# Other shares of the stores of output chunks 0 to 2 among the DMA engines

## The reference, cut to what matters

```python
kv = einsum('bhsd,bhse->bhde', k, v); out = einsum('bhsd,bhde->bhse', q, kv)
x = out / sqrt(mean(out * out, -1) + 1e-06) * g_norm      # -> 4608 tokens x 512
logits = x @ phi                                          # 4608 x 32 slots
d = softmax(logits over tokens); slot_input = d.T @ x     # 32 x 512
slot_out[e] = relu(slot_input[e] @ w1[e]) @ w2[e]         # 8 experts, 4 slots each
c = softmax(logits over slots); result = c @ slot_out     # 4608 x 512, float32
```

## Time and profile before

| | us |
|---|---|
| time, median of 3 runs | 171.68 (171.65 to 171.72) |
| the profiled execution's own time | 171.66 |
| its span | 170.3 |
| TensorE busy | 150.0 (88%) |
| ScalarE, VectorE busy | 88.4, 86.7 |
| GpSimd busy | 59.6 |
| packets of SP's transfers, share of 16 DMA engines' span | 97.9% |

### The profile page before, as it was taken

One profiled execution on the slowest core, in us unless ns is written; L12 is line 12 of the kernel. 1 busy time (PEld: TensorE's weight loads), 2 busy tenths in 40 slices (PEclk: granted clock), 3 DMA queues, 4 the chain that ended last, 5 costly groups with the idle time before them and its releaser, 6 DMA issues.

```text
span 170.3 us, 4236 instructions
## 1 busy us (share of the span) xinstructions
PE 150.0 (88%) x1834; PEld 103.8 (61%) x1834; DVE 86.7 (51%) x185; ACT 88.4 (52%) x230; POOL 59.6 (35%) x73
## 2 busy tenths in 40 slices
PE   7978999989999899999899998989999989989200
PEld 3546878979688888796697674345665533545000
DVE  1111427483687265762946798824888136318300
ACT  3005768796975987759749864202224034417300
POOL 7000246848357755367482679400000004000000
PEclk9999999999999999999999999999999999999955
DMA  5999999999999999999999999999999999999997
GB/s 182 440 439 414 439 421 435 475 417 457 450 411 409 458 429 416 435 400 460 400 466 392 452 408 418 443 446 406 431 427 439 437 450 389 410 423 442 430 424 312
DMA packets 4077, 71.65 MB, mean 421 GB/s; under 512 B 758, under 2 KB 758, under 8 KB 890
## 3 DMA queue, kind: packets, MB, share of 16 engines
q1 hardware_dynamic: 3706, 71.18, 97.9%
q0 software_dynamic: 352, 0.20, 0.4%
HBM read 61.94 MB, written 9.44 MB: 419 GB/s over the span
## 4 chain that ended last, share of the span: by engine, by line
PE 56%; DMA 16%; ACT 14%; DVE 6%; issue 1%; SPq 0%
PE psum L215 56%; DMA arena<-in_w_dram 10%; DMA arena<-in_kv_dram 6%; ACT bd L215 4%; ACT sq L215 4%; ACT xall L215 2%; DVE logits L215 1%; DVE ms L215 1%; ACT part L215 1%; ACT arena L215 1%; ACT d L215 1%; DVE part L215 1%; ACT r L215 1%; DVE acc L215 1%; DVE r L215 0%
## 5 line engine op out<-in xcount | busy, mean ns | idle before, releaser
L215 PE MATMUL psum<-bd,arena 128*128 128x192 f32 (+1 forms) x320 | 56.1, 335 | 2.1 <-ACT bd L215 1.5
L215 PEld LDWEIGHTS psum<-bd,arena 128*128 128x128 f32 (+1 forms) x320 | 45.4, 179 | 9.0 <-ACT bd L215 2.8
L215 DVE TENSOR_REDUCE ms<-sq 128x16 f32<-128x1024 f32 (+1 forms) x19 | 22.1, 1162 | 30.5 <-ACT sq L215 30.4
L215 POOL TENSOR_TENSOR part<-part,r 128x512 f32<-128x512 f32 x17 | 17.8, 1047 | 49.1 <-DVE r L215 49.1
L215 POOL TENSOR_TENSOR xall<-xall,r 128x512 f32<-128x512 f32 x34 | 34.7, 1042 | 0.0
L215 ACT ACTIVATE sq<-psum 128x512 f32<-128x512 f32 x36 | 21.4, 595 | 10.6 <-PE psum L215 10.5
L215 PEld LDWEIGHTS psum<-arena 128*64 128x64 f32 (+1 forms) x640 | 18.8, 137 | 7.1 <-issue 3.0
L215 PE MATMUL psum<-arena 128*64 128x64 f32 (+1 forms) x640 | 21.5, 226 | 1.3 <-DMA arena<-in_kv_dram 1.0
L215 ACT COPY xall<-psum 128x512 f32<-128x512 f32 x34 | 20.6, 607 | 0.0
L215 ACT COPY part<-psum 128x256 f32<-128x256 f32 (+1 forms) x38 | 13.6, 359 | 9.1 <-DVE part L215 8.0
L215 DVE TENSOR_REDUCE logits<-part 128x64 f32<-128x512 f32 (+1 forms) x18 | 17.8, 987 | 0.0
(11 more groups left out here) (80 smaller groups left out, 128.8 us busy)
## 6 DMA issues: line engine op xcount, KB each, us to landing
arena<-in_w_dram SPq DMA_DIRECT2D x4, 4096.0 KB, 23.8
arena<-in_w_dram SPq DMA_DIRECT2D x4, 2048.0 KB, 20.4
arena<-in_kv_dram SPq DMA_DIRECT2D x3, 2304.0 KB, 21.6
arena<-in_t_dram SPq DMA_DIRECT2D x1, 6912.0 KB, 36.1
arena<-in_w_dram SPq DMA_DIRECT2D x2, 3072.0 KB, 22.8
arena<-in_kv_dram SPq DMA_DIRECT2D x1, 4608.0 KB, 40.3
arena<-in_kv_dram SPq DMA_DIRECT2D x1, 3584.0 KB, 29.9
out_dram<-arena SPq DMA_DIRECT2D x1, 3072.0 KB, 10.7
```

The lines of the kernel that those rows point to most:

```text
L215: inst = getattr(engine, method)(*args, **kwargs)
```

## The change

Only the list `FIRST` changes.

```diff
 FIRST = (
-    ("sync", 1, 4, 30, 5, 1, 0, 1), ("sync", 121, 4, 2, 3, 3, 0, 1),
-    ("gpsimd", 1, 4, 24, 2, 1, 1, 2), ("gpsimd", 97, 4, 8, 2, 1, 1, 2),
-    ("sync", 3, 4, 32, 1, 1, 0, 2), ("sync", 0, 2, 64, 1, 1, 0, 3), ("sync", 1, 2, 64, 1, 1, 2, 3),
+    ("sync", 1, 4, 28, 7, 1, 0, 1), ("sync", 113, 4, 4, 3, 3, 0, 1),
+    ("gpsimd", 1, 4, 22, 2, 1, 1, 2), ("gpsimd", 89, 4, 10, 3, 3, 1, 2),
+    ("sync", 0, 2, 64, 1, 1, 0, 3), ("sync", 3, 4, 32, 1, 1, 0, 3),
+    ("sync", 5, 8, 14, 7, 1, 2, 3), ("sync", 117, 8, 2, 1, 1, 2, 3), ("sync", 1, 8, 16, 1, 1, 2, 3),
 )
```

## The result

The changed kernel is slower: 172.23 us (171.6 to 172.77, 22 runs) against 171.74 (171.59 to 171.94, 22 runs) for the kernel before on the same chips; ratio 1.0027, 95% interval 1.0018 to 1.0035. Its fastest run is as fast as the kernel before, but its runs spread over 1.2 us, those of before over 0.35: six took 171.94 us or less, six 172.5 or more, and ten lie between, from 172.07 to 172.39. The profiled execution took 172.74 us, at the upper end of these runs.

A forecast was written before the change was run, and what follows sets the result against it. The DMA engine finishing last was taken to bound the kernel. Shared rows -0.24, empties +0.15 and own shares moved the last end from 169.93 to 169.91 us, so 171.68 - 0.02 = 171.66 us; range 171.4 to 171.95.

The forecast's parts named there:

- The ends of the streams: Last-store marks before the change, assigned to streams: 15 first at 168.12 us, the last at 169.93, mean 169.43.
- step 4: Sum of the parts per stream: 5 and 6 end last at 169.91 us instead of 169.93, so -0.02.
- Common rows, -0.24: Rows that all sixteen engines share, regrouped: 4.32 us per engine instead of 4.56.
- POOL's queue: Empty packets in POOL's queue: 45 packets per engine instead of 20, +0.15 us for every engine.
- 30 x 0.080: Stream 15's own share: thirty 2 KB pieces from POOL replace four of 6 KB, +1.48 us, ending at 169.4.
- Step 6: Rows carried by engines that otherwise serve other rows: packet prices unchanged, cost 0; stream 15 has no delay of its own.
- Issue: SP issues five transfers in a row behind chunk 2, from 143.1 to 146.0 us; no engine waits, cost 0.
- Stream 1 is not the late one: Rival on streams 1 to 4: stream 1 is the one ending last, +0.15 us, giving 171.83; 15%.
- The shares fall otherwise: Rival on stream numbering: pieces land where they even the ends more, up to -0.59 us, 171.1; 9%.
- POOL's pieces go over ten engines: Rival on POOL's 30 pieces: three on each of engines 0 to 9, +0.06 us, 171.74; 6%.
- An instruction load is added: Rival: SP's longer list brings one more q14 load onto a late stream, +0.3 to 0.8 us there, 172.2; 6%.
- the 2% rival: POOL's second store: pieces starting after 167.8 us would push the end out by 0.34 us; 2%.

The follow-up runs named there:

- e4: The changed kernel run again, unchanged, for another profile: 172.62 us, ratio 1.0043 to the kernel before; its profiled execution took 171.69.
- e1: Kernel before with only the rows that all sixteen engines share regrouped: 171.85 us, ratio 1.0004.
- e11: The changed kernel, unchanged, one run as the third of a batch: 171.89 us.
- e14: The changed kernel once more, unchanged, for one more profile: 172.54 us (3 runs), ratio 1.0053 to the kernel before.
- e2: e1 plus the change's 6 KB pieces on engines 5 and 6, POOL's stores as before: 172.69 us, ratio 1.0043 to the kernel before.
- e9: e2 once more, unchanged, one run as the first of a batch: 171.63 us.
- e12: e2 again, unchanged, for a slow execution: 172.04 us, ratio 1.0019 to the kernel before; its profile is the run of 172.67.
- e3: e1 plus POOL's stores as in the change (ten rows in 2 KB pieces), no share for 5 and 6: 172.29 us, ratio 1.0022.
- e13: e3 with eight rows instead of ten in POOL's 2 KB pieces, SP storing the other two on engines 0 and 1: 171.87 us, ratio 1.0005.
- e5: e3 with nine rows in 3 KB pieces on engine 15 instead of ten in 2 KB, SP storing three rows: 171.79 us, ratio 1.0002.
- e15: e5 with eleven rows instead of nine in 3 KB pieces on engine 15: 172.19 us (6 runs), ratio 1.0037.

## Why the prediction was wrong

*What bounds the kernel.* Right: the last DMA engine, and the end of the marks moved by what the time moved. That an even spread can bring at most 0.50 us was hardly tried; nothing speaks against it, as no kernel here came under 0.9995.

*The ends of the streams.* Here it failed. I wrote "5 and 6 at 168.53 and 168.61" and "Eight streams have them, six of these twice", and took the one execution's places for the program's. The eight streams and the 1.42 us are right, but which two have one load only changes. With two on 5 and 6 step 4 would have read 168.61 + 1.42 + 1.39 - 0.09 = 171.33 (measured 170.99), and with 171.66 - 169.93 = 1.73 behind the last end 173.06 for the time (measured 172.74); with one it reads 169.91 and 171.66, the forecast, and e4, which had one, measured 171.69. The kernel before hides this: 5 and 6 with two loads would end at 170.03 there, and the regrouped e1 has them at 169.71, with its time unchanged. Their 1.3 us in hand were no slack; they were the room for a load that comes in other executions.

*Common rows, -0.24.* The streams 9 to 14 with two loads in the profile of 171.69 (e4) agree in sign and roughly in size: they end by 169.62, against 169.92, where -0.24 and the +0.06 of the next point make -0.18. e1 leaves this term at 0 and only shows that the new grouping is free (1.0004).

*POOL's queue.* "Every engine gets as many packets as the one with most data, empties included" is right, but not the count: two 2 KB pieces make one packet. Packets on q0 that start from 140 us to the end, after:

```profile
q0 software_dynamic: 480, 0.20, 2.5%
```

So 30 per engine, (11+1) + (1+1) + (15+1), not 45, beside 20 before: +0.06 us and not +0.15.

*Stream 15: "30 x 0.080".* Mis-sized, and the second place where one execution was taken for all. I expected 169.4; measured are 170.42, 169.94 (e4), 170.05 (e11) and 170.00 (e14). A packet of 4 KB takes 0.159 us where nothing holds it up, so fifteen take what I priced. In the profile of 172.74 only six of the fifteen do; nine take longer, 1.11 us in all. The one that starts in 151.784 to 151.79 us, with one mark:

```profile
q0 software_dynamic: 2, 0.00, 541.7%
```

is 5.417 x 16 x 0.006 - 0.009 = 0.51 us. In e4, where only two are held up (0.35 and 0.27 us), one that starts in 153.07 to 153.08 us:

```profile
q0 software_dynamic: 1, 0.00, 99.4%
```

takes 0.159. Step 6 put "so 0" here, from packets of before that were on time; that did not carry over. Nor is it a matter of the 2 KB pieces: with 24 KB from POOL stream 15 ended at 168.12 (before), 168.74 (e1), 169.90 (e2), 168.54 (e9) and 168.02 (e12). By step 4 the change would end it at 169.90 + 1.48 - 0.24 = 171.14 in an execution like that of e2 (an estimate; no profile shows one). I set aside the rule of the Trainium skill, DMA: Bandwidth & Descriptors, "Latency and other measured facts", that DMA engines 7 and 15 are usually slower, because the trace of before did not agree. The runs do, in part: stream 15 lost over 0.3 us to held-up packets in thirteen of the sixteen profiles with a store by POOL, and one of 7 and 8 lost 0.86 in e1. But they also lie on 1 (e14) and on one of 2 to 4 (e11), where the rule has nothing. The runs do not show the cause that the Trainium skill proposes there.

*Issue.* Right, no gap.

*Rivals.* Stream 1 is not the late one of 1 to 4: the streams with a piece more in e2 are 0 and 1, and neither is it. "The shares fall otherwise" and "POOL's pieces go over ten engines" fell: one stream alone has the 4 KB packets. "An instruction load is added" had the right cause, a load on a stream that ends late, but not as it happens: q8 has fourteen and q14 five as before; they only fall elsewhere. Late pieces of POOL's second store, the 2% rival, did not come: the last starts at 153.86 us in the profile of 172.74.

Open: what decides where the round of instruction loads starts; what holds packets up, on 15 most often, but also on 0, 1, one of 2 to 4, 7 or 8, and 9 to 14; and the executions of e3 between 172.3 and 172.6 and of the changed kernel between 172.07 and 172.39, of which there is no profile. The median of the changed kernel, 172.23, is one of these, so what makes it is argued and not seen. A late stream 15 fits: in the profile of 172.74 the time is 1.75 us behind the last end, and with 5 and 6 on time its stream 15 would have given 170.42 + 1.75 = 172.17 (an estimate). e13, e5 and e15, where the time follows the bytes on stream 15, say the same.

## What to carry to other kernels

Where the DMA engines are full to the end, the room of the engines that end early is real only if it is there in every execution. Follow the engines through several profiles of the same kernel before giving them bytes; a spread of the changed kernel's runs that is wider than that of the kernel before is the sign that something which moves has come onto the critical path. Shares for such engines have to be cut for their worst case: this kernel's 5 and 6 have none to give, and of the 1.8 us of stream 15 an execution like that of e2 leaves nothing.

## What the runs showed of the hardware

- A program's large instruction loads (fourteen of 16 KB here) go round eight of the sixteen DMA engines and cost the engine 1.42 us each (the median over the seventeen profiles). Where the round starts changed between executions of one program: 5 and 6 had one load each in e4 and two each in e14. Two starts were seen, four places apart. The small ones (q14, five of 8 KB) came onto the same three engines in every profile.
- POOL's transfers put a packet on every engine for each packet of the busiest one, empties included: 480 packets in all for 192 KB (above), 320 for 192 KB before.
- Pieces of 2 KB and of 3 KB that POOL stored travelled two to a packet; SP's 2 KB pieces travelled singly (0.084 us).
- Packets on a full engine can be held up: one of 6 KB took 0.95 us (e2), 0.88 (e11) and 0.78 (e14) instead of 0.234, one of 16 KB 1.21 instead of 0.611 (e1). Stream 15, with the same share in each, lost 2.0 us so in e2 and nothing in the kernel before.
